# Attention, expert layer and gated product on one core: the attention's steps put into another sequence on every engine

## The reference

```
scores = q @ k.T / sqrt(64) + min(-(cum_i - cum_j), 0)   # masked above the diagonal
attn   = softmax(scores);   x = attn @ v                 # -> (1152, 512)
P      = exp(x @ w_gate - max);  8 times: P /= row sums; P /= column sums; P *= N / E
y      = sum_e P[:, e] * (relu(x @ w1[e]) @ w2[e])       # 8 experts, 512 -> 1024 -> 512
out    = ((y @ w_a) * (y @ w_b)) @ w_out                 # 512 -> 1536 -> 512
```

## Time and profile before

| | |
|---|---|
| timed, median of 3 runs | 1208.78 us (1207.66 to 1210.09) |
| profiled execution | 1206.97 us |
| its span, first to last instruction | 1205.0 us |
| TensorE busy | 1165.5 us, 97% |
| TensorE weight loads | 1040.4 us, 86% |
| VectorE, ScalarE, GpSimd busy | 411.9, 289.9, 43.1 us |
| mean granted clock of TensorE | 0.984 of full |

### The profile page before, as it was taken

The page is one execution under the profiler, slowest core; times in us unless marked ns, Lnnn a source line. Parts: engine busy times, 40 slices in busy tenths (PEclk is TensorE's granted clock), DMA queues, the critical chain, the costliest instruction groups (busy, mean ns, idle before and its releaser), DMA issues.

```text
span 1205.0 us, 15622 instructions
## 1 busy us (share of the span) xinstructions
PE 1165.5 (97%) x6314; PEld 1040.4 (86%) x6314; DVE 411.9 (34%) x800; ACT 289.9 (24%) x587; POOL 43.1 (4%) x47
## 2 busy tenths in 40 slices
PE   7878789999999999999999999999999999999998
PEld 5555579989998998998998999899899899999997
DVE  6445433433132322413313322232241333433422
ACT  4444432022121220311312212031131222232221
POOL 2222103000000000000000000000000000000000
PEclk8888999999999999999999999999999999999999
DMA  8324122021011102202201110120220110120101
GB/s 221 72 64 108 48 71 71 1 70 54 18 35 53 52 4 65 70 0 70 70 0 52 52 35 18 51 70 0 70 70 1 35 44 28 36 71 1 35 27 53
DMA packets 52537, 59.14 MB, mean 49 GB/s; under 512 B 31600, under 2 KB 31600, under 8 KB 52496
## 3 DMA queue, kind: packets, MB, share of 16 engines
q1 hardware_dynamic: 51296, 58.27, 16.8%
q10 hardware_dynamic: 1200, 0.30, 0.1%
HBM read 56.15 MB, written 2.40 MB: 49 GB/s over the span
## 4 chain that ended last, share of the span: by engine, by line
PE 86%; DVE 0%; issue 0%; ACT 0%; ACTq 0%
PE bank L1173 15%; PE bank L1174 15%; PE bank L1175 15%; PE bank L1320 13%; PE bank L1321 13%; PE bank L1322 13%; PE bank L1259 1%; PE bank L1158 0%; PE bank L1332 0%; PE bank L1120 0%; PE bank L1132 0%; PE bank L1297 0%; ACT pT L469 0%; ACT hh L569 0%; PE bank L1267 0%
## 5 line engine op out<-in xcount | busy, mean ns | idle before, releaser
L1173 PE MATMUL bank<-xh,w1h 128*128 128x384 f32 x1056 | 354.5, 336 | 0.0
L1175 PE MATMUL bank<-xh,w1l 128*128 128x384 f32 x1056 | 353.0, 334 | 0.0
L1174 PE MATMUL bank<-xl,w1h 128*128 128x384 f32 x1056 | 352.9, 334 | 0.0
L1320 PE MATMUL bank<-w2h,hh 128*128 128x512 f32 x684 | 267.1, 390 | 0.0
L1322 PE MATMUL bank<-w2h,hl 128*128 128x512 f32 x684 | 266.3, 389 | 0.0
L1321 PE MATMUL bank<-w2l,hh 128*128 128x512 f32 x684 | 266.2, 389 | 0.0
L569 ACT ACTIVATE hh<-bank 128x384 fp32r<-128x384 f32 x192 | 94.4, 492 | 617.1 <-PE bank L1175 617.1
L1173 PEld LDWEIGHTS bank<-xh,w1h 128*128 128x128 f32 x1056 | 198.2, 188 | 1.3 <-issue 0.2
L1174 PEld LDWEIGHTS bank<-xl,w1h 128*128 128x128 f32 x1056 | 198.3, 188 | 0.7
L1175 PEld LDWEIGHTS bank<-xh,w1l 128*128 128x128 f32 x1056 | 198.2, 188 | 0.0
L777 DVE SCALAR_TENSOR_TENSOR hl<-bank,hh 128x384 fp32r<-128x384 f32 x192 | 106.8, 556 | 250.7 <-ACT hh L569 250.7
(11 more groups left out here) (113 smaller groups left out, 565.4 us busy)
## 6 DMA issues: line engine op xcount, KB each, us to landing
stage<-in_moe_w SPq DMA_DIRECT2D x64, 512.0 KB, 3.5
bias<-cum_dram SPq DMA_DIRECT2D x14, 256.0 KB, 3.5
stage<-in_moe_w_a SPq DMA_DIRECT2D x12, 256.0 KB, 2.7
stage<-in_moe_w_b SPq DMA_DIRECT2D x12, 256.0 KB, 3.1
stage<-in_moe_w_out SPq DMA_DIRECT2D x12, 256.0 KB, 2.5
bias_tail<-cum_dram SPq DMA_DIRECT2D x16, 144.0 KB, 4.2
nat<-in_q SPq DMA_DIRECT2D x16, 128.0 KB, 4.1
vt<-in_v SPq DMA_DIRECT2D x16, 128.0 KB, 2.4
```

Of the source, the lines that this page charges most:

```text
L1173: pe.matmul(o, w1h[:, c, col:col + PART], high, start=(c == 0), stop=False)
L1174: pe.matmul(o, w1h[:, c, col:col + PART], low, start=False, stop=False)
L1175: ins = pe.matmul(o, w1l[:, c, col:col + PART], high, start=False, stop=(c == KC - 1))
L1320: pe.matmul(o, hh[:, n % 2, f, at], w2h[:, f, :], start=(f == 0), stop=False)
```

## The change

The loops of TensorE, VectorE, ScalarE and GpSimd now run over periods k from -1 to 10 instead of pairs, and each step has its own lag: a period holds, for example, the second attend of pair k-2, the scores of pair k, the P transposes of pair k-1 in the order 2, 3, 1, 6, 7, 4, 5, unit 0 of pair k itself, and the transposes of q and k of pair k+1. Steps of a pair that isn't there are left out by `present`. The tail's scores are split into two steps, `score_tail(p, 0)` and `(p, 1)`. Copies are shared anew: ScalarE takes units 3, 1, 7, 4 (it had 3, 5, 7), VectorE 0, 2, 6, 5 (it had 0, 1, 2, 4, 6). The order of the biased scores and of the exps changes. Of the six expert groups, 0 to 2 stand in period 8 and 3 to 5 in period 10. On SP `load_bias` comes before `load_v`. Four more warm-up matmuls are issued. `group_bank` is rotated by two. The work that each step does is the same.

The core of the diff, added lines above all (the loops that it takes out are in the listing above):

```diff
@@ -23,7 +23,7 @@
 PART = 128
 EPS = 1e-9
 SINKHORN_ROUNDS = 8
-WARM_UP = 7
+WARM_UP = 11
...
-    RING = [("tail", 0), ("tail", 1)]
...
+    PERIODS = range(-1, PAIRS + 3)
+    def present(p):
+        return 0 <= p < PAIRS
...
+    RING = []
+    for _k in PERIODS:
+        RING += [step for step in (("unit", _k - 1, 2), ("tail", _k), ("unit", _k - 1, 3), ("unit", _k - 1, 1),
+                                   ("spread", _k - 1, 0), ("unit", _k - 1, 6), ("unit", _k - 1, 7),
+                                   ("unit", _k - 1, 4), ("unit", _k - 1, 5), ("spread", _k - 1, 1),
+                                   ("unit", _k, 0)) if present(step[1])]
...
+    UNIT_NTH = {0: 1, 2: 2, 3: 3, 1: 4, 6: 5, 7: 6, 4: 7, 5: 8}
+    BY_DVE = {0: 1, 2: 2, 6: 3, 5: 4}
+    BY_ACT = {3: 1, 1: 2, 7: 3, 4: 4}
+    BIASED_NTH = {(0, 0): 1, (1, 1): 2, (1, 0): 3, (0, 1): 4, (2, 0): 5, (2, 1): 6, (3, 1): 7, (3, 0): 8}
+    EXP_NTH = {(0, 0): 1, (0, 1): 2, (1, 1): 3, (2, 1): 4, (2, 0): 5, (1, 0): 6, (3, 1): 7, (3, 0): 8}
...
-    BY_DVE = {0: 1, 1: 2, 2: 3, 4: 4, 6: 5}
-    BY_ACT = {3: 1, 5: 2, 7: 3}
...
-        return (FC * n + f) % len(L1_BANK)
+        return (FC * n + f + 2) % len(L1_BANK)
...
@@ -370,10 +378,9 @@
         for p in range(PAIRS):
             if p + 2 < PAIRS:
                 load_qk(p + 2)
+                load_bias(p + 2)
             if 2 <= p + 1 < PAIRS:
                 load_v(p + 1)
-            if p + 2 < PAIRS:
-                load_bias(p + 2)
...
-            if p > 1:
-                low_x(p - 2, 1)
-            if 1 <= p <= PIECES:
-                split_w1_first(p - 1)
-            if p > 0:
-                low_x(p - 1, 0)
-            if p + 1 < PAIRS:
-                spread_tail_queries(p + 1)
-        low_x(PAIRS - 2, 1)
-        low_x(PAIRS - 1, 0)
-        low_x(PAIRS - 1, 1)
+        for k in PERIODS:
+            low_x(k - 3, 1)
+            spread_tail_queries(k)
+            if 0 <= k - 2 < PIECES:
+                split_w1_first(k - 2)
+            low_x(k - 2, 0)
...
+            act.wait_ge(sc_done, 10 * p + BIASED_NTH[t, r])
+            if (t, r) == (0, 0):
+                at_least(act, eps_done, p - 1)
...
         def copy_pT(p, u):
-            act.wait_ge(pt_mm, 8 * p + u + 1)
-            at_least(act, pv_mm[1], p)
+            if not present(p):
+                return
+            act.wait_ge(pt_mm, 8 * p + UNIT_NTH[u])
+            at_least(act, pv_mm[0 if u < 2 else 1], p)
             bank = ring_bank("unit", p, u)
-            if u == 3:
-                copy(pT[:, 1, 0:3, 2 * PART:3 * PART], bank[:, 0:3 * PART].rearrange("p (j s) -> p j s", j=3), pt_act)
-            elif u == 5:
-                copy(pT[:, 1, 0:4, 3 * PART:MAIN], bank[:, :].rearrange("p (j s) -> p j s", j=4), pt_act)
+            if u == 1:
+                dst, src = pT[:, :, 0:2, PART:2 * PART], bank[:, :].rearrange("p (r j s) -> p r j s", r=2, j=2)
+            elif u == 3:
+                dst, src = pT[:, 1, 0:3, 2 * PART:3 * PART], bank[:, 0:3 * PART].rearrange("p (j s) -> p j s", j=3)
+            elif u == 4:
+                dst, src = pT[:, 0, 0:4, 3 * PART:MAIN], bank[:, :].rearrange("p (j s) -> p j s", j=4)
             else:
-                copy(pT[:, :, FULL, MAIN:S], bank[:, 0:PART].rearrange("p (r s) -> p r s", r=2), pt_act)
+                dst, src = pT[:, :, FULL, MAIN:S], bank[:, 0:PART].rearrange("p (r s) -> p r s", r=2)
+            copy(dst, src, pt_act)
...
+        for k in PERIODS:
+            copy_pT(k - 1, 1)
+            exp_tile(k, 0, 0)
+            high_qk(k + 1, 0)
+            if k == PAIRS:
+                high_hidden(0, 0, 0)
+            exp_tile(k, 0, 1)
+            copy_spread(k - 1, 0)
+            high_qk(k + 1, 1)
+            if k == -1:
+                first_bias_rows()
+            if k == PAIRS + 1:
+                high_hidden(0, 0, 2)
+            high_x(k - 2, 0)
+            copy_pT(k - 1, 7)
+            high_x(k - 2, 1)
+            copy_pT(k - 1, 4)
+            if k == PAIRS + 1:
+                high_hidden(0, 0, 3)
+            exp_tile(k, 1, 1)
+            exp_tile(k, 2, 1)
+            if k == PAIRS + 1:
+                high_hidden(0, 0, 4)
+            if k == PAIRS:
+                high_hidden(0, 0, 1)
+            exp_tile(k, 2, 0)
+            exp_tile(k, 1, 0)
+            if k == PAIRS + 2:
+                high_hidden(0, 0, 5)
+            copy_spread(k - 1, 1)
+            exp_tile(k, 3, 1)
+            exp_tile(k, 3, 0)
+            high_qk(k + 1, 2)
+            exp_tail(k)
+            copy_pT(k, 3)
+            if k == 4:
                 act.wait_ge(gate_loaded, DMA)
                 act.wait_ge(zero_set, 4)
                 copy(wgh[:, :, 0:E], wgf[:, :, :], wg_hi)
-        def high_hidden(e, n, f):
-            group = FC * (NB * e + n) + f
-            act.wait_ge(l1_mm, group + 1)
-            act.activation(hh[:, n % 2, f, :], L1_BANK[group_bank(n, f)][:, 0:BLK], ACT.Relu).then_inc(h_hi, 1)
-        def high_w2(e, i):
...
+            if (t, r) in ((0, 0), (2, 0), (3, 1)):
+                dve.wait_ge(sc_mm, 5 * p + max(t, 1))
+            if p == 0:
+                dve.wait_ge(first_bias, r + 1)
+            elif (t, r) == (0, 0):
+                at_least(dve, pt_mm, 8 * (p - 1))
+                dve.wait_ge(bias_loaded[z], DMA * (4 * (p // 2 + 1) - (2 if z == 0 else 0)))
+            dve.tensor_tensor_reduce(scores[z][:, r, COL[t]:COL[t + 1]], bank[:, col:col + n], bias[z][:, r, 0:n],
...
+        for k in PERIODS:
+            low_qk(k + 1, 0)
+            copy_pT(k - 1, 5)
+            low_qk(k + 1, 1)
+            biased(k, 3, 1)
+            if k == PAIRS + 1:
+                low_hidden(0, 0, 2)
+            scale_x(k - 1, 0)
+            if k == PAIRS + 2:
+                low_hidden(0, 0, 3)
+            copy_pT(k, 0)
+            biased(k, 3, 0)
+            biased_tail(k, 0)
+            if k == PAIRS:
+                low_hidden(0, 0, 0)
+            biased_tail(k, 1)
+            copy_pT(k, 2)
+            low_qk(k + 1, 2)
+            biased(k + 1, 0, 0)
+            if k == PAIRS:
+                low_hidden(0, 0, 1)
+            biased(k + 1, 1, 1)
+            add_eps(k)
+            invert(k)
+            scale_x(k - 1, 1)
+            biased(k + 1, 1, 0)
+            if k == PAIRS + 2:
+                low_hidden(0, 0, 4)
+            biased(k + 1, 0, 1)
+            biased(k + 1, 2, 0)
+            if k == PAIRS + 2:
+                low_hidden(0, 0, 5)
+            biased(k + 1, 2, 1)
+            copy_pT(k, 6)
+            if k == 4:
                 dve.wait_ge(wg_hi, 1)
...
-                    ins.then_inc(sc_mm, 1)
+        def score_tail(p, half):
+            if not present(p):
+                return
+            z = p % 2
+            pe.wait_ge(bd_done, p + 1)
+            pe.wait_ge(sc_done, 10 * p + BIASED_NTH[2, half])
+            if p == 0:
+                pe.wait_ge(const_set, 5)
+            for i, (a, b) in enumerate(TERMS):
+                ins = pe.matmul(S_BANK[2 + half][:, 0:HALF], bd[z][:, a, :],
+                                qk[z][:, b, 1, half * HALF:(half + 1) * HALF], start=(i == 0),
+                                stop=(i == 2 and half == 0))
+            if half == 1:
+                ins = pe.matmul(S_BANK[3][:, MAIN - HALF:HALF], identb[:, :], maskt[:, :], start=False, stop=True)
+            ins.then_inc(sc_mm, 1)
...
                 blocks = [(r, u, j) for r in range(2) for j in range(u + 1)]
             elif u < 6:
                 t, r = divmod(u + 2, 2)
-                pe.wait_ge(exp_done, 9 * p + u + 3)
+                needs = [(t, r)]
                 blocks = [(r, t, j) for j in range(t + 1)]
             else:
-                pe.wait_ge(exp_done, 9 * p + 9)
+                needs = []
                 blocks = [(None, FULL, j) for j in (range(FULL) if u == 6 else [FULL])]
+            pe.wait_ge(exp_done, 9 * p + (max(EXP_NTH[tile] for tile in needs) if needs else 9))
...
@@ -1140,11 +1148,14 @@
             ins.then_inc(spread_mm, 1)
         def attend(p, g):
+            if not present(p):
+                return
             z = p % 2
             lo, hi = QRANGE[g]
             if g == 0:
                 pe.wait_ge(v_loaded[z], 3 * DMA * (p // 2 + 1))
-                pe.wait_ge(pt_dve, len(BY_DVE) * p + 2)
+                pe.wait_ge(pt_dve, len(BY_DVE) * p + BY_DVE[0])
+                pe.wait_ge(pt_act, len(BY_ACT) * p + BY_ACT[1])
             else:
                 pe.wait_ge(pt_dve, len(BY_DVE) * (p + 1))
                 pe.wait_ge(pt_act, len(BY_ACT) * (p + 1))
...
+        def spread_first_bias():
+            pe.wait_ge(cum_done, 1)
+            for r in range(2):
+                pe.matmul(S_BANK[2 + r][:, :], ident[0:HEADS, r:r + 1].broadcast_to([HEADS, PART]),
+                          cum_rows[:, 0:MAIN], start=True, stop=True).then_inc(first_bias_mm, 1)
+        for k in PERIODS:
+            attend(k - 2, 1)
```

(81 more changed lines are left out.)

220 lines of the change are left out of this document (24 added, 196 removed).

## The result

The changed kernel takes 1160.32 us (median of four runs, 1158.92 to 1160.68) against 1209.43 us for the kernel before, measured beside it: a ratio of 0.9589 [0.9568, 0.9611]. The profiled execution took 1158.92 us against 1206.97. The gain is 48 to 49 us.

What follows compares the result with a forecast made beforehand. Bound: copy latency in a fixed order, and the clock falls behind those waits, before the gate. Ceiling 41.6 us, less 3.2 of waits and 3.5 for one fall, gives 34.9 us gain: 1173.9 us, 8 in 10 range 1165 to 1189.

Steps and rivals of the forecast that it cites:

- the narrowest (unit 7 to unit 5): Two-bank ring in the attention turn: 0.9 us of cover for unit 7's 128-column copy, at least 0.2 us to spare.
- the walk: Attention turn in the new order, step costs added from differences of starts: unit 0 at 12.9 us, no wait left.
- TensorE floor of 14.0 us: One turn of the attention loop over pairs: TensorE's busy time at full clock, taken as the least a turn can last.
- ceiling: Stage before the gating matmuls: 158.5 us could fall to 116.9 without waits and turns' half clock, at most 41.6 us gained.
- The allowances: Attention stage: 0.4 us of waits left per turn, 3.2 over eight, and one clock fall of 3.5 us.
- The clock term: Attention turns: half clock in three slow turns and the last costs 11.9 us, to go with the waits.
- The clock follows the waits: Attention stage: TensorE's clock falls behind long waits; a wait makes a fall likely and not certain.
- The rule on transposes: Attention stage: the skill says full clock does not engage for transposes, so it might stay slow even without waits.
- The rival that rested on it: Attention held at half clock by its mix of transposes and half-array matmuls: gain -24 us, 1232 us; 4%.
- A long wait in each turn: Attention turns: another late copy, 8 x 1.47 = 11.8 us, plus three clock falls, 10.6; 1189.6 us; 12%.
- The rival that the clock falls all the same: Attention: a fall in every turn, 7 x 3.5 = 24.5 us, and 3.2 of waits; gain 13.9, 1195 us; 8%.
- the one of late inputs: Attention: inputs of later pairs arrive at the old pace, so no change, 1208.8 us; 2%.

Runs made afterwards that it cites:

- two swaps: Kernel before, ScalarE's unit 5 copy put ahead of the tail's exp and VectorE's unit 2 copy ahead of biased tile 2: 1176.75 us, 0.9721.
- the first swap: Kernel before, only ScalarE's copy of unit 5 put ahead of the tail's exp: 1186.82 us, 0.981.
- 1.88 us a turn: Changed kernel, ScalarE's copy of unit 4 put behind five exps, so the second spread waits: 1180.52 us, 0.9754.
- the one tried: Kernel before with both copies moved ahead (ScalarE unit 5, VectorE unit 2), plus second attend behind the next turn's first q transposes: 1177.33 us, 0.9719.
- Seven warm-ups with the early load: Changed kernel, q and k of pair 2 loaded ahead of w1 and gate weights, seven warm-up matmuls instead of eleven: 1153.21 us, 0.9526.
- the early load: q and k of pair 2 loaded ahead of w1 and gate weights: changed kernel (eleven warm-ups) 1151.29 us, 0.9514; kernel before 1206.95 us, 0.9971.

## Why the prediction was wrong in size and right in kind

**Right.** What bounded the attention stage was order and not load: no work was removed, the copies' sharing brought nothing, and the late copies that I named, taken ahead one by one, gave 24 and 10 us. None of the waits I said would go stayed, none of those I feared came: no wait before a spread, turns at clock 1.00, the last stage at 1021. The extra warm-ups cost nothing under the wait for the load, which stayed near 25.6 (25.09), and the DMA share became 0.44 (forecast 0.43). Of the margins, the narrowest (unit 7 to unit 5) was given as 0.2 us at the least. In the timeline of the kernel after, unit 7's copy ends at 71.87, and unit 5's transposes, four behind 71.80 at 0.1 each, begin at 72.2: 0.3. The walk's 0.15 us from the start of the last matmul to its end was too little, 0.28 by the row of unit 7's transpose, but the copy behind it, 0.28 too, was shorter than the walk allowed.

```profile
71.28 0.28 PE L1126 MATMUL bank<-ident,scores_tail 128*128 128x128 f32 x1
...
71.59 0.28 ACT L472 ACTIVATE pT<-bank 128x128 f32<-128x128 f32 x1 [0.76 <-PE bank L1126]
71.80 1.03 PE L1126 MATMUL bank<-ident,scores 128*128 128x128 f32 x8
```

**The step that failed: the sum's floor, "TensorE floor of 14.0 us".** I took it from the busy time of the turns at full clock. The new turn takes 13.19 us. The walk in the same prediction, made of differences of starts, put unit 0 at 12.9 and so the turn's end at about 13.2; it was right, and I summed with the other number. Where the sum had 116.9 us for the stage rid of all waits and falls, the stage took 111.0, and it began 0.5 us earlier: 6.4 of the missing 13.1 us, about eight turns at 0.8, and the reason why the "ceiling" of 41.6 was none. For the old order the 116.9 was good: with two swaps TensorE was busy for 117.24 us of the stage. There waits went and the busy time of a turn stayed at 14.00. So the 0.8 goes with the old order, and most likely with its short waits, which the modelled ends of matmuls cover. Two places, in the timeline of the kernel before, each with six transposes of the same kind:

```profile
67.51 0.82 PE L1120 MATMUL bank<-ident,scores 128*128 128x128 f32 x6
...
69.79 1.14 PE L1120 MATMUL bank<-ident,scores 128*128 128x128 f32 x6
```

and the weight loads of the second, which do show the waits:

```profile
69.78 0.31 PEld L1120 LDWEIGHTS bank<-ident,scores 128*128 128x128 f32 x3 [0.31 <-DVE pT L762]
...
70.38 0.31 PEld L1120 LDWEIGHTS bank<-ident,scores 128*128 128x128 f32 x3 [0.29 <-DVE pT L762]
```

Six transposes take 0.3 us more where a bank had to come free in between, and the matmul row has no bracket for it. In the new order eight in a row take 1.03. With such places in each turn, five of them above for the run with two swaps, the 0.8 is accounted for in kind; that they add up to just 0.8 is not shown.

**The allowances.** I left 0.4 us of waits a turn (3.2 us) and one fall of the clock (3.5). Neither occurred in the attention's turns. With the 6.4 above that is 13.1, the whole difference between 34.9 and 48.0. The two allowances, 6.7 us, missed by as much as the floor did; but my range allowed for them, down to 1165, and not for the floor.

**Point by point.** The gate at 136.11 against "142 to 150" and turns of 13.2 against "14 to 15" are the same error. The clock term, 11.9, is borne out by the 12.3 us of busy time that went with the first swap. The four more warm-up matmuls took 1.1 us and not 1.9: the timelines have the 22 records of the kernel after end at 5.72, and the 14 of the kernel before at 4.67. "The clock follows the waits" is shown in both directions; "likely and not certain" remains, since the kernel before had two full-clock turns among its six.

**The rule on transposes.** The turn from 62.22 has 35 transposes of P, q and k among its 124 matmuls, up to 11 of them side by side where it had been 10, and its granted clock is 1.00 as in every turn after 35.85. The Trainium skill (TensorE: Matmul & The Clock Gate, Part 4: PE-mode transpose) says that full clock does not engage for transposes, which would have kept the attention from it; here the measurement decides against it. The rival that rested on it, the attention at half clock, would have given 1232 us.

**The other rivals.** A long wait in each turn did not occur, but was made: at 1.88 us a turn the time is 20 us worse, against the 22.4 that the rival priced for 1.47 and three falls. The rival that the clock falls all the same and the one of late inputs show nothing in the trace.

**Open.** With two swaps 16 to 18 us of gain remain that no single further move gave; the one tried only moved a wait. How they divide among the many moves of the full change was not taken apart. What makes one long wait bring a fall and the next one none is open too.

**Seven warm-ups with the early load** cost 1.9 us by the medians and not the 3 to 4 that I expected, and the runs of the two overlap (1152.32 to 1154.59 and 1150.26 to 1153.93). In its trace TensorE comes to q of pair 2 at 20.33 us instead of 17.54, 2.8 later, and 0.4 of it goes into the wait that the run with eleven has for q of pair 3. The 3 to 4 us rested on a start at half speed as in the kernel before; in that trace it begins at full speed (last section).

## What to carry to other kernels

Take an engine's floor from differences of starts where it never waits, not from its busy time, and look at the weight loads' waits for those that the matmuls' records cover; walk each in-order engine's new queue and sum by that walk. Try the one swap that ends the longest wait first: it gave half, since the clock came back with it, while moving one more step only moved a wait. When a stage is rid of its waits, look next at the load it starts with: here its order was worth 9 us, for a few lines, and in the old order, where other waits took its place, some 3.5 us.

## What the runs showed of the hardware

**The clock fell behind long idle stretches.** In the profiled execution with one swap, idle stretches of 1.47, 0.7 and 0.4 us stood in each turn of 16.7 us, and TensorE kept 2.4 GHz; with a single one of 1.88 us in a turn of 15.1 it was granted 1.2 GHz for a part of four turns in a row (0.90 in their windows). In the kernel before the stretches were 1.77 and 1.47, and four turns of six had falls. The first of these turns idles 16% of its time by the records and the second 12%, so the idle share of a turn did not tell which would fall. That it is the longest stretch that tells fits these traces and is no more than a guess from few turns: two turns of the kernel before and two of the run with 1.88 us kept full clock with the same stretches.

**At the start the clock column and the durations disagree.** The timelines of TensorE at the start, before and then after, for the same four bias matmuls:

```profile
8.45 3.77 PE L1194 MATMUL bank<-cum_rows,ident 16*128 16x512 f32 x4
```
```profile
7.20 1.98 PE L1205 MATMUL bank<-cum_rows,ident 16*128 16x512 f32 x4
```

They take 3.77 us and 1.98: half speed behind seven warm-ups, full speed behind eleven. Yet the window of the kernel before that holds most of the slow ones reads 1.00:

```profile
8.00:12.00 4.00, 4.00 (x7) 1.44 (x6) 1.51 (x3) 1.36 (x3) 0.72 (x1) 1.00 0.57 153
```

In the first microseconds the durations are to be trusted. Nor do seven warm-ups always mean half speed. In the trace with the early load and seven of them the eight transposes of q took 1.06 us, where they took 1.94 in the kernel before, and the bias matmuls behind them 2.58, so the speed fell partway through these; the window from 8 to 12 us reads 0.55 there.

```profile
6.14 1.06 PE L1028 MATMUL bank<-ident,nat 128*128 128x128 f32 x8 [1.47 <-DMA nat<-in_q]
7.13 2.58 PE L1207 MATMUL bank<-cum_rows,ident 16*128 16x512 f32 x4
```

In these traces four more warm-ups bring full speed to the whole of the first real work, 1.8 us in this one group, which can show in the time only once the load behind it is early too.

**A small VectorE instruction stretched beside GpSimd.** VectorE's addition over 128x9 values, 0.16 us at the median, took 2.18 us where it started 0.2 us behind a GpSimd subtraction of 2.35 us, and both ended within 0.03 us of each other; in the kernel before it took 2.17 us in the same place. What holds it was not tested.
